# Output by rows of tokens in the first MLP's down layer, with the activations as the stationary operand

## What is computed

```python
def _moe_ref(x, w_ch1, w_ch2):
    X = np.fft.fft(np.fft.fft(x, axis=1), axis=2)
    u = x + np.real(X)
    un = (u - mean(u)) / np.sqrt(var(u) + 1e-6)
    ch = np.maximum(un @ w_ch1, 0.0) @ w_ch2
    return u + ch                      # called x2 below

def _moe2_ref(x, U, V, w_ch1, w_ch2):
    u = x + ((x^T @ U) @ V)^T
    return u + np.maximum(u @ w_ch1, 0.0) @ w_ch2
```

## Time and profile before

| what | value |
|---|---|
| median of 3 runs | 1857.5 us (1851.31 to 1861.46) |
| profiled execution | 1865.05 us, span 1862.7 us |
| busy share of the span | PE 94%, PEld 90%, DVE 75%, ACT 42%, POOL 32% |
| group 0, up and down half start | 271.4 and 349.5 us |
| groups 1 to 4 | 428.2 to 944.5 us, 129.1 us each |
| groups 5 and 6 end | 1075.5 and 1226.5 us |
| groups 7 to 10 | 127.6 to 127.8 us each |
| group 11 ends | 1858.4 us |

### The profile page before, as it was taken

One profiled execution on the slowest core, in us unless ns is written; L12 is line 12 of the kernel. 1 busy time (PEld: TensorE's weight loads), 2 busy tenths in 40 slices (PEclk: granted clock), 3 DMA queues, 4 the chain that ended last, 5 costly groups with the idle time before them and its releaser, 6 DMA issues.

```text
span 1862.7 us, 25843 instructions
## 1 busy us (share of the span) xinstructions
PE 1752.5 (94%) x9908; PEld 1681.7 (90%) x9908; DVE 1387.9 (75%) x1559; ACT 783.9 (42%) x1126; POOL 604.2 (32%) x428
## 2 busy tenths in 40 slices
PE   5989868979999999999999999799999999999998
PEld 5767758969999999999999999789999999999998
DVE  3899975897797787877866768965956857758667
ACT  1333333634443544544444436334334434443442
POOL 2888862453041231330320213620410402303203
PEclk9999988989999999999999999899999999999999
DMA  7557548898688787787876778786676766766663
GB/s 251 182 196 237 195 155 315 307 336 295 246 299 273 258 298 270 280 290 257 295 257 232 255 244 316 285 299 221 247 241 232 240 234 245 249 226 240 228 247 122
DMA packets 123819, 470.04 MB, mean 252 GB/s; under 512 B 12273, under 2 KB 49649, under 8 KB 84018
## 3 DMA queue, kind: packets, MB, share of 16 engines
q1 hardware_dynamic: 122482, 467.21, 71.1%
q10 hardware_dynamic: 1216, 1.18, 0.2%
HBM read 389.70 MB, written 78.64 MB: 251 GB/s over the span
## 4 chain that ended last, share of the span: by engine, by line
PE 72%; DVE 15%; issue 5%; POOL 3%; DMA 3%; SPq 0%; ACT 0%; ACTq 0%; DVEq 0%; POOLq 0%
PE pair L837 11%; PE pair L839 11%; PE pair L838 11%; PE pair L854 11%; PE pair L856 11%; PE pair L855 10%; DVE t_raw L1366 3%; DVE t_lo L1347 2%; PE tr_ps L721 2%; DMA in_sb<-x_dram 1%; POOL x_sb L1527 1%; DVE eo_sb L1238 1%; DVE ce_sb L1246 1%; PE pair L628 1%; DVE ss_sb L1212 1%
## 5 line engine op out<-in xcount | busy, mean ns | idle before, releaser
L854 PE MATMUL pair<-t_hi,w_sb 128*128 128x384 f32 x1344 | 462.8, 344 | 33.8 <-DVE t_lo L1347 33.7
L837 PE MATMUL pair<-t_hi,w_sb 128*128 128x384 f32 x1344 | 462.4, 344 | 15.6 <-DVE h_sb L1384 8.3
L855 PE MATMUL pair<-t_lo,w_sb 128*128 128x384 f32 x1344 | 458.2, 341 | 0.0
L856 PE MATMUL pair<-t_hi,w_sb 128*128 128x384 f32 x1344 | 458.1, 341 | 0.0
L838 PE MATMUL pair<-t_lo,w_sb 128*128 128x384 f32 x1344 | 457.3, 340 | 0.0
L839 PE MATMUL pair<-t_hi,w_sb 128*128 128x384 f32 x1344 | 457.2, 340 | 0.0
L1347 DVE TENSOR_TENSOR t_lo<-t_raw,t_hi 128x768 fp32r<-128x768 f32 x300 | 346.4, 1162 | 11.0 <-ACT t_hi L1067 7.6
L1572 POOL TENSOR_TENSOR t_raw<-h_sb 128x768 f32<-128x768 f32 x60 | 150.4, 2507 | 573.7 <-PE pair L856 573.7
L1082 ACT ACTIVATE t_hi<-t_raw 128x768 fp32r<-128x768 f32 x240 | 202.1, 846 | 314.9 <-DVE t_raw L1366 236.4
L854 PEld LDWEIGHTS pair<-t_hi,w_sb 128*128 128x128 f32 x1344 | 254.6, 189 | 42.6 <-DVE t_lo L1347 42.3
L837 PEld LDWEIGHTS pair<-t_hi,w_sb 128*128 128x128 f32 x1344 | 254.0, 189 | 23.7 <-issue 14.1
(11 more groups left out here) (149 smaller groups left out, 2115.8 us busy)
## 6 DMA issues: line engine op xcount, KB each, us to landing
w_sb<-wc SPq DMA_DIRECT2D x260, 1024.0 KB, 4.9
wc<-w_sb SPq DMA_DIRECT2D x28, 1024.0 KB, 5.8
w_raw<-wr1a SPq DMA_DIRECT2D x24, 512.0 KB, 4.9
w_raw<-wr1b SPq DMA_DIRECT2D x24, 512.0 KB, 4.2
wc<-pb SPq DMA_DIRECT2D x16, 640.0 KB, 4.8
w_raw<-wr2a SPq DMA_DIRECT2D x10, 1024.0 KB, 7.0
wc<-pb_v SPq DMA_DIRECT2D x16, 640.0 KB, 4.8
w_raw<-wr2b SPq DMA_DIRECT2D x10, 1024.0 KB, 7.2
```

Source lines behind the costliest of these rows:

```text
L837: nc.tensor.matmul(ps, w_hi, hi[:, x, :], start=(fresh and x == 0), stop=False, skip_group_check=True)
L854: nc.tensor.matmul(ps, w_hi, hi[:, f, :], start=(fresh and k == 0 and f == 0), stop=False, skip_group_check=True)
L855: nc.tensor.matmul(ps, w_hi, lo[:, f, :], start=False, stop=False, skip_group_check=True)
L856: last = nc.tensor.matmul(ps, w_lo, hi[:, f, :], start=False, stop=(k == 3 and f == 1), skip_group_check=True)
```

## The change

In groups 0 to 5 the two operands of a down matmul change places. The stationary operand is now 128 tokens of the activations, the moving one the weights of 256 output features. A step has 18 matmuls of 256 columns where it had 12 of 384, and the output lies by rows of tokens: three blocks of 128 tokens by 256 features, 768 columns in a row of the same pair of banks. No transposes follow, and no `add_residual`.

The residual is loaded into `res_sb`, now one tensor in the memory of `ch_sb`, before the products are read: at steps 26, 28 and 30. The reads of the first MLP follow the scheme of the second: the shared sum (in the new `share_sb`), products 4 and 3 added by VectorE to the residual, the shared sum added to the residual's diagonal blocks by GpSimd at step 41, products 7 and 6 added by VectorE. x2 is split, gathered and stored from `res_sb` at the steps of before.

```diff
 def dn_step(g, i, k):
+                if g < NS:
+                    for f in range(2):
+                        w_hi, w_lo = w[:, 0, 2 * (k % 2) + f, :, :], w[:, 1, 2 * (k % 2) + f, :, :]
+                        for c in range(CH):
+                            ps = pair[DN_PAIR[i]][:, 256 * c:256 * (c + 1)]
+                            cols = slice(128 * c, 128 * (c + 1))
+                            nc.tensor.matmul(ps, hi[:, f, cols], w_hi, start=(fresh and k == 0 and f == 0 and c != 1), stop=False,
+                                             skip_group_check=True)
+                            nc.tensor.matmul(ps, hi[:, f, cols], w_lo, start=False, stop=False, skip_group_check=True)
+                            last = nc.tensor.matmul(ps, lo[:, f, cols], w_hi, start=False, stop=(k == 3 and f == 1),
+                                                    skip_group_check=True)
+                    last.then_inc(step, 1)
+                    return
...
-                        if t in OUT_AT:
-                            tr_free(g, "out", NCH * (g - 1) + OUT_AT.index(t))
-                            turn_out(g - 1, OUT_AT.index(t))
...
+    res_sb = at("res_sb", a0 + 49152, [128, NCH, D])
+    share_sb = at("share_sb", base + 57344, [128, CH, 2 * 128])
...
-                    if g < NS and t in (44, 48, 52):
-                        load_res(g, (t - 44) // 2)
-                        load_res(g, (t - 44) // 2 + 1)
+                    if g < NS and t in (26, 28, 30):
+                        load_res(g, t - 26)
+                        load_res(g, t - 25)
...
-                elif name == "d4":
-                    act.wait_ge(step, step_done(g, "dn", 4, 3))
-                    nc.scalar.activation(ch_block("21"), both(DN_PAIR[4]), ACT.Copy).then_inc(act_read, 1)
...
+                    if name in ("d7", "d6"):
+                        dve.wait_ge(v_ready, 2 * (g + 1))
+                    elif g < NS:
+                        residual_there(dve, g, block)
...
+                    if g < NS:
+                        total, added = res_block(block), res_block(block)
+                    else:
+                        total, added = ch_block(block), a_block(g, block)
+                    nc.vector.tensor_tensor(total, product(g, i), added, ALU.add).then_inc(dve_read, 1)
...
-            def add_residual(g, j):
-                n = NCH * g + j
-                dve.wait_ge(out_turned, n + 1)
-                dve.wait_ge(res_loaded[j], 16 * (g + 1))
-                nc.vector.tensor_tensor(res_sb[j][:, :], tr_ps[:, :], res_sb[j][:, :], ALU.add).then_inc(x2_ready, 1)
...
             def add_first(g, block):
                 pool.wait_ge(dve_read, dve_count(g, "d1"))
-                nc.gpsimd.tensor_tensor(a_block(g, block), a_block(g, block), ch_block("22"), ALU.add).then_inc(v_ready, 1)
+                if g < NS:
+                    residual_there(pool, g, block)
+                total = res_block(block) if g < NS else a_block(g, block)
+                nc.gpsimd.tensor_tensor(total, total, shared(g), ALU.add).then_inc(v_ready, 1)
...
-                    if g >= NS and t == 41:
+                    if t == 41:
                         add_first(g, "11")
                         add_first(g, "22")
```

More of the change, by code:

```diff
@@ L295, in both, with rows, shared, product @@
             return pair[n][:, :].rearrange("p (t n) -> p t n", t=2)[:, :, 0:TILE]
+        def rows(n):
+            return pair[n][:, 0:CH * 256].rearrange("p (c n) -> p c n", c=CH)
+        def shared(g):
+            return ch_block("22") if g >= NS else share_sb[:, :, :]
+        def product(g, i):
+            return (rows if g < NS else both)(DN_PAIR[i])
         def sem(name):
@@ L376, in raw_made, with x2_there, residual_there @@
             return pool, dve
+        def x2_there(engine, g, j):
+            engine.wait_ge(dve_read, dve_count(g, "d7" if j < CH else "d6"))
+        def residual_there(engine, g, block):
+            for j in range(CH):
+                engine.wait_ge(res_loaded[CH * (int(block[1]) - 1) + j], 16 * (g + 1))
         def sides(g, e):
@@ L869, in tr_free @@
                 first = q % NCH == 0
[L870 to L874, removed]
-                elif what == "mix":
+                if what == "mix":
                     if g > NS:
@@ L879, in tr_free @@
                         pe.wait_ge(in_ready, q)
-                    elif first:
-                        pe.wait_ge(x2_ready, NCH * g)
                     else:
@@ L888, in tr_free @@
                     pe.wait_ge(seq_copied, 8 * B)
-                elif first and g < NS:
-                    pe.wait_ge(x2_ready, NCH * g)
                 else:
@@ L1045, in take_in @@
                         act.wait_ge(gathered, NCH * NS)
-                        for r in range(4):
-                            act.wait_ge(x2_stored[r], 16 * NS)
                     else:
@@ L1112, in read @@
                     nc.scalar.activation(h_block("22", k), h_block("22", k), ACT.Relu).then_inc(act_read, 1)
[L1113 removed]
+                else:
                     act.wait_ge(step, step_done(g, "dn", 2, 3))
[L1115 to L1116 removed]
+                    if 1 <= g < NS:
+                        act.wait_ge(v_ready, 2 * g)
+                    elif g == NS:
+                        act.wait_ge(x2_lo_ready, NCH * NS)
+                        for j in range(NCH):
+                            act.wait_ge(x2_stored[j], 16 * NS)
                     elif g > NS:
                         act.wait_ge(out_stored["22"], 16 * (g - NS))
[L1119 to L1125 removed]
+                    nc.scalar.activation(shared(g), product(g, 2), ACT.Copy, scale=-1.0).then_inc(act_read, 1)
             def split_x2_hi(g, j):
                 n = NCH * g + j
[L1129 removed]
+                x2_there(act, g, j)
                 if n:
                     act.wait_ge(gathered, n)
[L1132 removed]
+                nc.scalar.activation(x2_hi[:, :], res_sb[:, j, :], ACT.Copy).then_inc(x2_hi_ready, 1)
             def turn_gathered(P):
@@ L1158, in _ @@
                         hi_up(g, 3)
-                    for at, name, k in act_events(g):
+                    for at, name, k in ACT_EV:
                         if at == t:
@@ L1391, in read @@
                     dve.wait_ge(act_read, act_count(g, "d2"))
-                    nc.vector.tensor_tensor(ch_block("22"), ch_block("22"), both(DN_PAIR[5]), ALU.subtract).then_inc(dve_read, 1)
+                    nc.vector.tensor_tensor(shared(g), shared(g), product(g, 5), ALU.subtract).then_inc(dve_read, 1)
                 elif name == "d1":
@@ L1459, in _ @@
                         lo_up(g, 4)
-                    for at, name, k in dve_events(g):
+                    for at, name, k in DVE_EV:
                         if at == t:
```

81 lines of the change are left out of this document (20 added, 61 removed).

## The result

The changed kernel takes 1868.9 us (median), the kernel before, run beside it, 1855.3 us. The ratio is 1.0062, with a 95% interval of 1.0048 to 1.0076: slower by 0.6%, or 11.5 us (8.9 to 14.1); the two medians by themselves are 13.5 us apart, inside that interval. The time lies inside the forecast's range, but the move is over twice the +4.5 us that the sum gave. The profiled execution of the changed kernel took 1868.74 us, with a span of 1866.9.

What follows compares the result with a forecast made beforehand. TensorE was taken to bound groups 1 to 4, VectorE group 0's down half. The terms -15.7 - 2.4 + 3.7 + 10.4 + 1.5 + 5.0 + 2.0 gave +4.5 us on 1857.5, so 1862 us, range 1846 to 1880.

Steps and rivals of the forecast that it cites:

- Turns, -15.7: Up halves of groups 1 to 6: 36 output blocks lose four transposes each, 0.436 us of TensorE per block, -15.7 us.
- Waits on line 1384, -2.4: Groups 1 to 4: TensorE's four waits for this PSUM reader each shrink by 0.60 us without the residual add, -2.4 us.
- Matmuls, +3.7: Down steps of groups 0 to 5: 18 matmuls at 0.119 us against 12 at 0.1767, over 168 steps, +3.7 us.
- The fixed price (0.1234): Rival, down matmuls: a fixed price each makes them 0.1234 us apart, +13.3 on the forecast, 1875 us; chance 0.15.
- the loads' floor (0.111): Rival, down matmuls: stationary loads set the pace at 0.111 us, -20.2 in place of +3.7, 1838 us; chance 0.04.
- the plain rate: Rival, down matmuls: 256 columns lose the faster rate, 0.217 us apart, a step 3.9 us, kernel 2157 us; chance 0.03.
- GpSimd's adds in groups 1 to 4, +10.4: Down halves: GpSimd's two adds lengthen three VectorE operations, so TensorE waits 2.6 us per group around steps 15 and 16, +10.4.
- Group 5, +1.5: Group 5: GpSimd's adds cost +1.5 us, as there is no split of a unit sum there, more like group 7.
- Group 0, +5.0: Group 0's down half, VectorE-bound: two operations lengthened by GpSimd's adds (3.3) and two VectorE adds (1.7), +5.0 us.
- Residual loads, +2.0 in group 0 and nothing in groups 1 to 5: Six loads moved ahead of weight loads on SP's queue: +2 us in group 0's full DMA stretch, nothing in groups 1 to 5.
- the third, waits twice as long in groups 1 to 4: Rival: two more VectorE operations held behind the unit sums, 5.6 us for 2.6 per group, +12, 1874 us; chance 0.10.

Runs made afterwards that it cites:

- the kernel with 384 columns: Changed kernel with 12 down matmuls of 384 columns, weights stationary, again in groups 0 to 5: groups 1 to 4 527.6 us against 527.2; one run 1878.0 us.
- late loads: Changed kernel with the residual loads of all six groups at steps 32 to 36: 1862.3 us, ratio 1.0027 to the kernel before.
- the kernel with VectorE's adds: Changed kernel with residual loads at steps 32 to 36 and groups 0 to 5's shared-sum adds on VectorE (steps 47, 51): 1851.9 us, ratio 0.9971.

## Why the prediction was right or wrong

1. **Turns, -15.7.** Right in groups 1 to 5: their up halves are 14.3 us shorter, of which 0.5 is the next point; five groups of six turns were 13.1. A turn weighed 0.46 us rather than 0.436: where one stood ahead of another row of transposes, the distance between matmuls fell from 1.32 to 0.86. Group 6's 2.6 didn't show in this profile (70.5 and 70.3 us): TensorE's wait on line 1384 there grew from 1.5 to 2.4 us. In seven of the nine other profiles without turns group 6's up half takes 67.9 to 68.5 us.
2. **Waits on line 1384, -2.4: wrong, -0.5** ( 2.6, now 2.1). VectorE's reader does come 0.6 us sooner. But the turn that went also brings TensorE there 0.46 us sooner, so each wait shrinks by 0.14 (0.65 to 0.51 or 0.52). The step counted a gain on both sides of one wait.
3. **Matmuls, +3.7: a little too high.** From 625.15 to 629.14 lie 34 distances at 256 columns, 0.117 us each:

```profile
625.15 0.28 PE L860 MATMUL pair<-w_sb,t_hi 128*128 128x256 f32 x1
...
629.14 0.28 PE L861 MATMUL pair<-w_sb,t_lo 128*128 128x256 f32 x1
```

   Over all of them the median is 0.118, so a step is 2.124 us against 2.120, +0.7 in all, and the kernel with 384 columns confirms it. The fixed price (0.1234), the loads' floor (0.111) and the plain rate are all excluded. The formula that the prediction takes from the Trainium skill, "TensorE: Matmul & The Clock Gate", section Back-to-back issue gap, is what that section gives as the gap of isolated matmuls, 0.109 at 256 columns; the stream here lies above it.
4. **GpSimd's adds in groups 1 to 4, +10.4: the mechanism right, the size too small**, 15.9 beside the moved loads and 14.5 with these out of the way (late loads). Two things were missed. The slack of 1.9, 2.3 and 1.0 us at steps 15, 16 and 17, read from the kernel before, is 0.9, 1.3 and 1.7 in group 2 once the loads alone have moved, and step 13, where it was 2.0, gets its low half 1.2 us late in the changed kernel. And even with late loads it isn't safe: in groups 2 and 3 the sums start 0.5 and 0.7 us later than before, and the low half of step 13 comes 0.1 us early. There the adds cost 4.3 us a group and not 2.6.
5. **Group 5, +1.5**: 1.6. **Group 0, +5.0**: the adds of GpSimd cost 4.7 by the kernel without them, where 3.3 was put; the two adds on VectorE, put at 1.7, didn't show: without GpSimd's adds its down half is 76.9 us, below the 78.7 of before. In all it rose by 2.8.
6. **Residual loads, +2.0 in group 0 and nothing in groups 1 to 5: the step that failed.** It was the other way round: 0.1 in group 0 and +6.2 in groups 1 to 4. The argument looked at the weight loads, seven slots ahead, and at SP's queue. It didn't look at the one other load of that stretch, the unit of step 30, for which GpSimd waits with nothing in hand. Nor is its lateness the price: the sums aren't urgent. They only move GpSimd's operands onto VectorE's operations.

Summed by what was measured: up halves of groups 1 to 5 -14.3, loads +6.2, adds 15.9 + 1.6, group 0's down half +2.8, make +12.2, and the measured change is 11.5. The nearest rival was the third, waits twice as long in groups 1 to 4 (1874): its 5.6 us per group is what the down halves show (5.5 to 5.8), and the row behind the unit sums does hold two more of VectorE's operations (639.31 and 645.26). What it had not seen is that the moved loads bring this about. (Two operations more are 3.3 us by the prediction's own rows, so its 5.6 should have read 5.9.)

## What to carry to other kernels

When loads are moved, list every transfer issued near the new place, and for each the engine that waits for it and what that engine runs into when it is late; "the queue is free" is no answer. A slack read before a change is worth nothing if another part of the change spends it first. And where GpSimd and VectorE share work on SBUF operands, an add of 0.95 us on the busy engine can be cheaper than one that the idle engine does beside it.

## What the runs showed of the hardware

- GpSimd and VectorE on SBUF operands: who starts first decides, and the loser's duration tells it. In the kernel with VectorE's adds GpSimd's operand of 916.38 took 4.85 us while VectorE's operations took 0.94 each, 0.87 apart; 8.5 us later GpSimd was first (2.31 us) and VectorE's took 2.60. So groups that run the same code differ: 129.0 us for group 1 there, 127.6 for group 3. The Trainium skill, "SBUF — State Buffer", section SBUF: two separate sides, says that whoever starts first gets the shared port pair for the whole instruction; the rows agree, and add that a row of VectorE's operations on SBUF operands can keep GpSimd out for several of them.
- The granted clock fell to half behind the longest waits of the changed kernel's groups 1 and 4, 2.24 us each (0.50 from 525.4 to 528.7, matmuls of 256 columns 0.213 us apart). Ahead of it TensorE had stood 1.35 and 2.24 us; groups 2 and 3 had 1.10 and 2.24 and kept the full clock, 2.4 GHz. The slower clock cost 0.3 us per group (131.9 and 132.0 against 131.6 and 131.7), for the wait ahead of step 16 went. The length of the stops alone doesn't tell the cases apart: with late loads the clock fell behind group 2's one stop of 2.20 us (0.50 from 650 to 652) and not behind group 3's of 2.21.
- A load of 512 KB issued directly behind two of 256 KB landed after 8.7 to 9.6 us (four loads of the changed kernel) and not 5.8 to 6.2 (the same four before), although the DMA engines' mean share over the four groups was 0.77, and 0.78 before. A share averaged over groups says nothing on a transfer that something waits for.
